# Rounding the second weight matrix on GpSimd instead of ScalarE, in a fused scan and expert kernel

## The reference

```python
sig = 1.0 / (1.0 + np.exp(-f_logit))
f = lower_bound[None, None, :] + (1.0 - lower_bound[None, None, :]) * sig
i = 1.0 - f
for t in range(S):
    h = f[:, t] * h + i[:, t] * x[:, t]
    y[:, t] = h
...
h = x @ w_in                       # (12160, 256) @ (256, 2048)
relu6 = np.clip(h + 3.0, 0.0, 6.0)
g = h * relu6 / 6.0
return (g @ w_out).astype(np.float32)   # (12160, 2048) @ (2048, 256)
```

## Time and profile before

| | us |
|---|---|
| median of 3 runs | 990.34 (989.96 to 990.44) |
| the profiled execution | 990.14 |
| its span | 988.1 |
| TensorE busy | 982.1 |
| VectorE busy | 817.4 |
| ScalarE busy | 715.0 |
| GpSimd busy | 204.1 |

### The profile page before, as it was taken

One profiled execution on the slowest core, in us unless ns is written; L12 is line 12 of the kernel. 1 busy time (PEld: TensorE's weight loads), 2 busy tenths in 40 slices (PEclk: granted clock), 3 DMA queues, 4 the chain that ended last, 5 costly groups with the idle time before them and its releaser, 6 DMA issues.

```text
span 988.1 us, 13020 instructions
## 1 busy us (share of the span) xinstructions
PE 982.1 (99%) x4372; PEld 817.8 (83%) x4372; DVE 817.4 (83%) x1186; ACT 715.0 (72%) x1215; POOL 204.1 (21%) x141
## 2 busy tenths in 40 slices
PE   8999999999999999999999999999999999999998
PEld 8988888888888888888888888888888888888887
DVE  7998987887888888888788788788878878886765
ACT  7777677777767767767777776777777777677665
POOL 2543131122104013111210401311121140131000
PEclk9999999999999999999999999999999999999999
DMA  7211001101102100110110210101011011001001
GB/s 245 86 59 65 22 22 43 64 23 42 65 1 64 43 22 24 56 50 22 43 65 1 65 43 22 52 35 43 22 43 64 4 61 43 1 1 43 1 0 43
DMA packets 17522, 42.38 MB, mean 43 GB/s; under 512 B 2480, under 2 KB 3760, under 8 KB 17456
## 3 DMA queue, kind: packets, MB, share of 16 engines
q1 hardware_dynamic: 17168, 41.42, 12.6%
q10 hardware_dynamic: 288, 0.13, 0.0%
HBM read 29.10 MB, written 12.45 MB: 42 GB/s over the span
## 4 chain that ended last, share of the span: by engine, by line
PE 98%; DMA 1%; DVE 0%; SPq 0%; ACT 0%; issue 0%; ACTq 0%
PE y_ps L1014 16%; PE y_ps L1012 16%; PE y_ps L1013 16%; PE x_ps L995 8%; PE x_ps L997 8%; PE x_ps L996 8%; PE v_ps L997 4%; PE v_ps L995 4%; PE v_ps L996 4%; PE z_ps L995 2%; PE z_ps L997 2%; PE z_ps L996 2%; PE x_ps L967 2%; PE y_ps L978 1%; PE y_ps L979 1%; PE y_ps L980 1%
## 5 line engine op out<-in xcount | busy, mean ns | idle before, releaser
L747 DVE TENSOR_TENSOR g_lo<-g,g_hi 128x512 fp32r<-128x512 f32 x352 | 273.3, 776 | 46.7 <-ACT g_hi L488 44.7
L1012 PE MATMUL y_ps<-g_hi,w_out_hi 128*128 128x512 f32 x704 | 273.9, 389 | 0.0
L1014 PE MATMUL y_ps<-g_hi,w_out_lo 128*128 128x512 f32 x704 | 273.9, 389 | 0.0
L1013 PE MATMUL y_ps<-g_lo,w_out_hi 128*128 128x512 f32 x704 | 273.9, 389 | 0.0
L488 ACT CAST g_hi<-g 128x512 fp32r<-128x512 f32 x352 | 210.1, 623 | 16.9 <-DVE g L742 16.6
L1013 PEld LDWEIGHTS y_ps<-g_lo,w_out_hi 128*128 128x128 f32 x704 | 132.1, 188 | 27.5
L1014 PEld LDWEIGHTS y_ps<-g_hi,w_out_lo 128*128 128x128 f32 x704 | 132.1, 188 | 27.5
L1012 PEld LDWEIGHTS y_ps<-g_hi,w_out_hi 128*128 128x128 f32 x704 | 132.1, 188 | 27.4
L479 ACT ACTIVATE g<-z_ps,half 128x512 f32<-128x512 f32 x88 | 60.8, 691 | 63.4 <-DVE z_ps L725 61.0
L479 ACT ACTIVATE g<-v_ps,half 128x512 f32<-128x512 f32 x88 | 60.7, 690 | 56.0 <-DVE v_ps L737 56.0
L731 DVE TENSOR_TENSOR h_sb<-v_ps,h_sb 128x512 f32<-128x512 f32 x88 | 60.9, 692 | 34.2 <-PE v_ps L997 32.9
(11 more groups left out here) (162 smaller groups left out, 1827.0 us busy)
## 6 DMA issues: line engine op xcount, KB each, us to landing
z_sb<-in_z SPq DMA_DIRECT2D x21, 512.0 KB, 3.6
x_sb<-in_x SPq DMA_DIRECT2D x21, 512.0 KB, 4.5
out_y<-y_sb SPq DMA_DIRECT2D x20, 512.0 KB, 3.1
w_out_raw<-in_w_out SPq DMA_DIRECT2D x8, 256.0 KB, 8.2
w_in_raw<-in_w_in SPq DMA_DIRECT2D x6, 256.0 KB, 6.7
z_sb<-in_z SPq DMA_DIRECT2D x2, 480.0 KB, 3.6
x_sb<-in_x SPq DMA_DIRECT2D x2, 480.0 KB, 4.1
out_y<-y_sb SPq DMA_DIRECT2D x3, 256.0 KB, 2.1
```

The lines of the kernel that those rows point to most:

```text
L747: nc.vector.tensor_tensor(g_lo[:, u], g[:, u], g_hi[:, u].bitcast(F32), ALU.subtract).then_inc(g_lo_ready[u], 1)
L1012: nc.tensor.matmul(out, w_out_hi[:, f, at], g_hi[:, u], start=opens, stop=False)
L1013: nc.tensor.matmul(out, w_out_hi[:, f, at], g_lo[:, u], start=False, stop=False)
L1014: return nc.tensor.matmul(out, w_out_lo[:, f, at], g_hi[:, u], start=False, stop=closes)
```

## The change

GpSimd gets a function of its own that rounds a block of w_out (a copy into the fp32r view), with the same wait on the block's load and the same semaphore behind it, and calls it in front of each rest. ScalarE's function and its eight calls go. Nothing else is touched.

```diff
+            def round_w_out(j):
+                pool.wait_ge(w_out_loaded[j], 16)
+                nc.gpsimd.tensor_copy(w_out_hi[:, pair(j)], w_out_raw[:, pair(j)]).then_inc(w_out_hi_ready, 1)
+
             def rest_of_w_out(j):
...
+            round_w_out(0)
             rest_of_w_out(0)
+            round_w_out(1)
             rest_of_w_out(1)
...
+            round_w_out(6)
             rest_of_w_out(6)
             rest_of_head_op(0)
             rest_of_head_op(1)
             make_s3(0)
+            round_w_out(7)
             rest_of_w_out(7)
...
-            def round_w_out(j):
-                act.wait_ge(w_out_loaded[j], 16)
-                nc.scalar.copy(w_out_hi[:, pair(j)], w_out_raw[:, pair(j)]).then_inc(w_out_hi_ready, 1)
...
             head_round_op(1)
-            round_w_out(0)
             round_w4(3)
...
-                if v == 0:
-                    round_w_out(1)
                 if v == 1:
-                    round_w_out(2)
                     round_w4(4)
...
-                if v == 13:
-                    round_w_out(7)
```

More of the change, by code:

```diff
@@ L380, in make_t4 @@
                                         ALU.subtract).then_inc(t4_ready, 1)
+            round_w_out(0)
             rest_of_w_out(0)
+            round_w_out(1)
             rest_of_w_out(1)
+            round_w_out(2)
             rest_of_w_out(2)
+            round_w_out(3)
             rest_of_w_out(3)
+            round_w_out(4)
             rest_of_w_out(4)
+            round_w_out(5)
             rest_of_w_out(5)
+            round_w_out(6)
             rest_of_w_out(6)
@@ L575, in _ @@
                 if v == 5:
-                    round_w_out(3)
                     head_gate(1, 1)
@@ L579, in _ @@
                     round_w4(6)
-                if v == 7:
-                    round_w_out(4)
                 if v == 8:
@@ L584, in _ @@
                 if v == 10:
-                    round_w_out(5)
                     head_round_op(2)
-                if v == 11:
-                    round_w_out(6)
                 if v == 12:
                     make_sig(0, 0)
-                if v == 13:
-                    round_w_out(7)
                 if v == 17:
```

## The result

The changed kernel takes 994.96 us (994.69 to 995.46 in four runs) against 990.39 for the kernel before in the same comparison: +4.57 us, ratio 1.0048, 95% interval 1.0037 to 1.0060. It is slower, as forecast, and inside the range. But the mechanism that I put first is not there; what took the time is the first rival, and it took about twice what I gave it.

The account below looks back on a forecast made before the run. TensorE was taken to bound the kernel. The later first down matmul (+6.55 us, library reload) and the clock's fall (+1.7) gave +8.25 us, other terms 0: 998.5 us, range 994 to 1001.5.

Parts of the forecast that it names:

- the mechanism that I put first: Before the first down matmul: a reload of 5 us or more behind GpSimd's first cast, in full on the path; chance 0.80.
- the first rival: GpSimd packed from 10.9 to about 33 us: free reload, collisions delay VectorE's g_lo; +2, 992.5 us; chance 0.05.
- What bounds the kernel: Whole span: TensorE, busy 982.1 of 988.1 us; early idleness is not won back; relief on ScalarE and VectorE taken as 0.
- The change is decided at 15.60 us: At TensorE's first down matmul, which waits for GpSimd's first rest of w_out and VectorE's g_lo, with everything queued behind it.
- The library reload, +6.55 us: Between GpSimd's first cast and first rest: reload taken as 8.9 us, moving the first down matmul from 15.60 to 22.15.
- the two rivals that built on it: Reload costs nothing visible and collisions decide (+2, chance 0.05); or not slower, reload at most 2.4 us (990.1, chance 0.08).
- The clock, +1.7: Behind the first down matmul: about 7.2 us of idleness drops TensorE to 1.2 GHz for a while; bounds 0 and 2.7.
- GpSimd's cast, 0.95 us: Each w_out block's cast on GpSimd takes 0.95 us, with bounds 0.6 and 1.3.
- During the wait VectorE works off what stands ahead: During TensorE's wait for the first down matmul VectorE and ScalarE gain several us of lead, so collisions cost 0.
- Faster at 0.01: Chance 0.01 of a faster kernel, since the change could touch only 0.6 us of TensorE's idle time in the head.

## Why the prediction was right in its time and wrong in its reason

- **What bounds the kernel**: right. TensorE is the end of everything, nothing lost early came back (from 40 to 100 us it is busy all 60.00 in both traces), and ScalarE's relief was worth nothing that shows: with casts spread, ScalarE's gain in full and the collisions only partly gone, the kernel is still 1.56 us slower.
- **"The change is decided at 15.60 us"**: wrong. That wait became shorter. The decision fell at 22.4, 26.1 and 29.2 us, in front of up products, at gates and not at rests of g.
- **The library reload, +6.55 us**: the step that failed. I bounded it by rows from 0 to 11.1 us and took 8.9, from transfers that seemed alike. Behind the first cast it measured nothing: 0.08 us to the rest, as where no reload stands; at the start it is under 0.82 us. That an instruction stands in the order and nothing is seen of it was read as a hidden cost; the rows allowed 0 as well, and that end should have had far more than the 0.13 of the two rivals that built on it. The Trainium skill's 6 us for the first call into a freshly loaded kernel (GPSIMD Engine Reference, section 2.1) are not paid here; whether because the library was already there the runs don't tell.
- **The clock, +1.7**: no stall of that length came about. The waits of 1.3 to 1.6 us did not lower the level (granted clock 1.00, and 0.17 to 0.18 us from start to start behind them), as the short one in the earlier trace rows had not. At the start of the program the pace of the earlier trace rows speaks for the lower level, but the profile gives a granted clock of 1.00 from 1.19 to 7.00 us too; the runs don't settle which it was.
- **GpSimd's cast, 0.95 us**: right in size, 0.80 to 1.07 in the trace, most near 0.94.
- **"During the wait VectorE works off what stands ahead"**: this made the collisions free in my sum, and it fell with the wait that it leaned on. A term put at nothing because another term hides it has to be priced again for the case that the other is zero. I did so in the first rival, with 0.05 of the chance.
- **First rival, +2 us**: right in kind, too small by 2.4 us. I counted only g_lo rows as able to collide, five more at 0.64 us. In the trace the weight rests (+0.40 and +1.09), a weight sum (+1.07), the drive (+0.35) and the scan (+0.36) collide too; with one g_lo (+0.63) that is 3.9 us of VectorE's time between the fourth gate and the seventh. The slack that I subtracted, about 1 us, was not there: 0.5 us at the first gate (2.22 us late, 1.72 lost), and none at the third, where gate and up product are both 4.00 us late. I had looked for slack at the rests of g (one ended at 28.01 and was wanted at 28.38) and not at the gates.
- **Faster at 0.01**: right; the one thing it could gain, 0.46 us of waiting at the first down product, it did gain, and it was worth nothing behind the gates.

The time of 998.5 was 3.5 us too high, since two terms of 8.25 us that don't exist stood in for one of about 4.4 that I had at nothing. That 994.96 lies inside 994 to 1001.5 is luck: the range was built from reloads of 5 us and more and from a fall of the clock, none of which happened, and the mechanism that did I had put at 992.5, outside it.

## What to carry to other kernels

Before work is moved to an engine because that engine is idle, ask what the two engines share: here GpSimd's idle 79% was the room in which VectorE's two-input operations ran undisturbed, and in the stretch from 14 to 30 us there was no slack to pay with (VectorE is busy for 16.81 of 17.00 us from 14 to 31 us). When work is taken up by an engine as soon as its data lands, it also comes earlier and denser than before; spreading it over the places where it was due took back two thirds of the loss without moving anything to another engine. An instruction that the profile shows no time for is to be given a chance of costing nothing that matches what the rows say, which here was no lower bound at all. Slack is to be read at every wait that the delay can reach: here it was 0.5 us at one gate and none two gates later.
